# Attention with a learned position bias and experts, one core: pass 0 in steps of 128 rows of two heads

## What is computed

```python
def _attn_ref(q, k, v, w1, b1, w2):
    scores = scale * np.matmul(q, k.transpose(0, 1, 3, 2))
    ...
    psi_rel = np.log1p(np.abs(rel))
    psi_i = np.log1p(np.maximum(pos[:, None].astype(np.float32), 1.0))
    x = (psi_rel / psi_i)[..., None]
    h = np.maximum(x @ w1 + b1, 0.0)
    bias = h @ w2
    scores = scores + bias.transpose(2, 0, 1)[None, :, :, :]
    ...
    attn = attn / (np.sum(attn, axis=-1, keepdims=True) + 1e-09)
    return np.matmul(attn, v).astype(np.float32)

def _moe_ref(x, domain_probs, w1, w2):
    p = domain_probs / (domain_probs.sum(-1, keepdims=True) + 1e-09)
    for e in range(E):
        h = np.maximum(x @ w1[e], 0.0)
        out += p[:, e:e + 1] * (h @ w2[e])
```

## Time and profile before

| | us |
|---|---|
| median of 3 runs | 617.83 (616.99 to 619.96) |
| the profiled run | 619.55 |
| its span in the profile | 617.8 |
| PE busy | 581.8 (94%) |
| DVE busy | 295.9 (48%) |
| ACT busy | 262.8 (43%) |
| POOL busy | 121.1 (20%) |
| mean DMA rate | 117 GB/s |

### The profile page before, as it was taken

The page is one execution under the profiler, slowest core; times in us unless marked ns, Lnnn a source line. Parts: engine busy times, 40 slices in busy tenths (PEclk is TensorE's granted clock), DMA queues, the critical chain, the costliest instruction groups (busy, mean ns, idle before and its releaser), DMA issues.

```text
span 617.8 us, 9792 instructions
## 1 busy us (share of the span) xinstructions
PE 581.8 (94%) x3864; PEld 468.3 (76%) x3864; DVE 295.9 (48%) x608; ACT 262.8 (43%) x506; POOL 121.1 (20%) x176
## 2 busy tenths in 40 slices
PE   3857998969999999999999999999999999999997
PEld 1336665636677888878888788998899889989986
DVE  6935567578546534464345624361255226224511
ACT  4755566457536544454336534352045015303400
POOL 5144689100001131334313321000000000000000
PEclk9977999979999999999999999999999999999999
DMA  4882665366455543283164401241223114222201
GB/s 145 218 293 85 192 193 150 105 176 201 117 183 175 169 131 92 65 237 110 40 193 124 125 22 55 99 138 34 69 81 124 35 35 138 67 69 55 83 35 51
DMA packets 60654, 72.72 MB, mean 118 GB/s; under 512 B 23232, under 2 KB 39872, under 8 KB 60608
## 3 DMA queue, kind: packets, MB, share of 16 engines
q1 hardware_dynamic: 60416, 72.08, 38.9%
q10 hardware_dynamic: 192, 0.01, 0.0%
HBM read 59.10 MB, written 12.98 MB: 117 GB/s over the span
## 4 chain that ended last, share of the span: by engine, by line
PE 82%; DVE 5%; ACT 5%; DMA 3%; issue 2%; POOL 2%; ACTq 0%; DVEq 0%; POOLq 0%
PE m_bank L1130 12%; PE scores L1113 11%; PE x_bank L1130 11%; PE scores L1130 10%; PE m_bank L1113 9%; PE x_bank L1113 9%; PE turn L1061 4%; PE scores L1032 4%; PE scores L1092 4%; PE scores L1000 3%; PE turn L1000 2%; ACT probs L894 1%; PE turn L1065 1%; ACT w_hi L916 1%; DVE w_lo L761 1%
## 5 line engine op out<-in xcount | busy, mean ns | idle before, releaser
L654 POOL TENSOR_SCALAR probs<-probs,recip 128x576 f32<-128x576 f32 x72 | 53.9, 759 | 241.1 <-DVE recip L745 240.9
L761 DVE TENSOR_TENSOR w_lo<-w_raw,w_hi 128x1024 fp32r<-128x1024 f32 x64 | 80.1, 1252 | 25.2 <-ACT w_hi L916 25.2
L730 DVE CUSTOM_DVE_ANT_0 probs<-scores,bias 128x576 f32<-128x576 f32 x72 | 51.9, 754 | 53.6 <-PE scores L1032 39.6
L900 ACT COPY probs_t<-turn 128x512 f32<-128x512 f32 (+2 forms) x80 | 42.4, 551 | 79.9 <-PE turn L1061 79.0
L916 ACT CAST w_hi<-w_raw 128x1024 fp32r<-128x1024 f32 x64 | 66.5, 1045 | 3.2 <-DMA w_raw<-w_in 3.2
L894 ACT ACTIVATE probs<-probs,neg_max 128x576 f32<-128x576 f32 x72 | 55.4, 771 | 28.6 <-DVE neg_max L730 28.1
L1061 PE MATMUL turn<-ident,probs 128*128 128x128 f32 x288 | 46.1, 292 | 5.6 <-POOL probs L654 4.8
L1113 PE MATMUL scores<-x_hi,w_hi 128*128 128x256 f32 (+2 forms) x152 | 49.7, 327 | 0.9 <-DVE w_lo L761 0.7
L1113 PE MATMUL scores<-x_lo,w_hi 128*128 128x256 f32 (+2 forms) x152 | 48.9, 322 | 0.0
L1113 PE MATMUL scores<-x_hi,w_lo 128*128 128x256 f32 (+2 forms) x152 | 48.9, 322 | 0.0
L1061 PEld LDWEIGHTS turn<-ident,probs 128*128 128x128 f32 x288 | 34.0, 146 | 15.5 <-POOL probs L654 7.6
(11 more groups left out here) (142 smaller groups left out, 1245.6 us busy)
## 6 DMA issues: line engine op xcount, KB each, us to landing
w_raw<-w_in SPq DMA_DIRECT2D x64, 512.0 KB, 3.6
qk_raw<-qk_t_in SPq DMA_DIRECT2D x16, 576.0 KB, 4.8
bias<-bias_scratch SPq DMA_DIRECT2D x16, 576.0 KB, 4.9
v<-v_in SPq DMA_DIRECT2D x32, 128.0 KB, 3.4
bias_scratch<-probs SPq DMA_DIRECT2D x13, 288.0 KB, 4.3
bias_scratch<-probs_t SPq DMA_DIRECT2D x10, 288.0 KB, 3.0
bias_scratch<-rows SPq DMA_DIRECT2D x8, 288.0 KB, 4.2
out_dram<-acc SPq DMA_DIRECT2D x8, 256.0 KB, 2.0
```

The costliest lines, as they stand in the source:

```text
L654: pool.tensor_scalar(tile, tile, recip[:, stat(f, p, j)], 1.0, ALU.mult, ALU.mult).then_inc(normed, 1)
L730: dve.tensor_tensor_reduce(probs_of(f, p, j).rearrange("p (c j) -> p c j", c=2), score_of(f, j)[:, :, 0:HALF], bias_of(f, p, j).rearrange( ...
L761: dve.tensor_tensor(lo, raw, hi.bitcast(F32), ALU.subtract).then_inc(w_lo_out, 1)
L900: act.copy(sub_out(f, p, i), sub_in(n, i)).then_inc(out_act, 1)
```

## The change

It rewrites pass 0 in steps. `ORDER0` becomes the first rows of pairs 0 to 3, then the second rows of pairs 0 to 3, then pair by pair from pair 4 on. Each step has three turns of its own (`TURNS` 6 for a pair): one tile of each head and then the last 64 columns of both; the first and the third are copied by ACT, the second by DVE. Products and x follow each step, with 128 columns, one step behind its turns; x_hi stands one step behind the turns on ACT and x_lo two on DVE, and the two halves of `x_banks` take turns. Four pairs have places for q, k and v: places 2 and 3 of q and k lie in parts of `x_hi` and `x_lo` that pass 1 fills later, and v has `v_more`. The early bias sums use the turn bank and `x_banks`, and their ring `rows` and `probs_t`. The scores of step 0 stand on PE before the last two early bias sums. SP's list and POOL's splits are in another order. Pass 1 and the experts are as before. The diff is cut here; changes that only rename or count are left out.

```diff
-TURNS = (5, 7)
+TURNS = (6, 7)
+PLACES0 = 4
...
-ORDER0 = [(0, 0), (1, 0), (0, 1), (1, 1)] + [(p, t) for p in range(2, PAIRS) for t in range(2)]
+ORDER0 = [(p, t) for t in range(2) for p in range(4)] + [(p, t) for p in range(4, PAIRS) for t in range(2)]
...
-PART_T = ((0, 3), (3, JT))
-PRODUCTS_AT = {5: [(0, 0), (0, 1)], 6: [(1, 0)], 7: [(1, 1)],
-               **{2 * p + 4 + part: [(p, part)] for p in range(2, PAIRS - 2) for part in range(2)},
-               STEPS: [(PAIRS - 2, 0), (PAIRS - 2, 1)]}
-X_AT = {s + 1: p for s, parts in PRODUCTS_AT.items() for p, part in parts if part == 1}
...
-ACT_TURNS = ((0, 2, 4), (0, 1, 2, 3, 4, 5, 6))
+ACT_TURNS = ((0, 2, 3, 5), (0, 1, 2, 3, 4, 5, 6))
...
-            return score_bank[n % 2] if n < EARLY else (score_bank[0], turn_bank)[n % 2]
+            return (turn_bank, x_banks)[n % 2] if n < EARLY else (score_bank[0], turn_bank)[n % 2]
...
                 for n in range(EARLY):
                     store_rows(n)
                     if n in (1, 3):
-                        load_v(0, n // 2)
-                    if n in (5, 8):
-                        load_raw(2 + n // 8)
-                    if n == 11:
+                        load_raw(2 + n // 2)
+                    if n in (4, 5):
+                        load_v(0, n - 4)
+                    if n == 10:
                         rows_all_stored(EARLY // 2)
                         load_bias0(0, 0)
+                        load_bias0(1, 0)
                 rows_all_stored(EARLY)
...
                 for s in range(STEPS + 1):
                     if s >= 1:
                         normalise(0, *ORDER0[s - 1])
-                    if s >= 3:
-                        g = 3 + (s - 3) // 2
+                    g = 3 if s in (1, 2) else 4 + (s - 5) // 2
+                    if s in (1, 2) or s >= 5:
                         if s % 2:
                             high_of_qk(g)
                         else:
...
-                    if s in X_AT:
-                        low_of_x(0, X_AT[s])
+                    if s >= LAG + 2:
+                        low_of_x(0, *ORDER0[s - LAG - 2])
                     if s >= LAG:
                         p, t = ORDER0[s - LAG]
-                        take_turn(0, p, 2 * t + 1)
+                        take_turn(0, p, 3 * t + 1)
...
-                    if s in X_AT:
-                        high_of_x(0, X_AT[s])
-                    if s >= LAG and t == 1:
-                        take_turn(0, p, 4)
+                    if s >= LAG:
+                        take_turn(0, p, 3 * t + 2)
+                    if s >= LAG + 1:
+                        high_of_x(0, *ORDER0[s - LAG - 1])
...
+                    if f == 0 and i % 3 == 2:
+                        for side in range(2):
+                            mm = pe.transpose(bank[0:J_LAST, P * side:P * side + P],
+                                              probs_of(0, p, 2 * (i // 3) + side)[:, 4 * P:S], ident[:, :])
...
+                def step(s):
+
+                    if 1 <= s < STEPS:
                         score_step(0, *ORDER0[s])
-                    if s >= LAG and s != LAG + 2:
-                        turns_of_step(*ORDER0[s - LAG])
-                    for p, part in PRODUCTS_AT.get(s, ()):
-                        products(0, p, part)
+                    if LAG <= s < STEPS + LAG:
+                        p, t = ORDER0[s - LAG]
+                        turn(0, p, 3 * t)
+                        turn(0, p, 3 * t + 1)
+                        turn(0, p, 3 * t + 2)
+                    if s >= LAG + 1:
+                        products(0, *ORDER0[s - LAG - 1])
+
+                pe.wait_ge(w2_steps, 1 + G)
+                for n in range(EARLY):
+                    sum_block(n)
+                    if n == EARLY - 3:
+                        pe.wait_ge(eye_in, 16)
+                        pe.wait_ge(cleared, CLEARED)
+                        score_step(0, *ORDER0[0])
+                for s in range(1, STEPS + 1):
+                    step(s)
```

More of the change, by code:

```diff
@@ L83, in turn_order @@
     for p, t in ORDER0:
-        order += [(0, p, 2 * t), (0, p, 2 * t + 1)] + [(0, p, 4)] * t
+        order += [(0, p, 3 * t + i) for i in range(3)]
     return order + [(1, p, i) for p in range(PAIRS) for i in range(TURNS[1])]
@@ L130, with taken_by, x_n @@
 TAKEN = turn_taken()
-def taken_by(f, p):
-    upto = TAKEN[:max(turn_n(f, p, i) for i in range(TURNS[f])) + 1]
+def taken_by(f, p, i):
+    upto = TAKEN[:turn_n(f, p, i) + 1]
     return sum(a for a, _ in upto), sum(not a for a, _ in upto)
+def x_n(f, p, t=0):
+    return STEP_N[p, t] if f == 0 else STEPS + p
 def chunk_order():
@@ L287, in attention_and_experts @@
         raw_in = [sem(f"raw_in{r}") for r in range(2)]
-        v_in = [sem(f"v_in{r}") for r in range(2)]
+        v_in = [sem(f"v_in{r}") for r in range(PLACES0)]
         bias0_in = [[sem(f"bias0_in{r}_{t}") for t in range(2)] for r in range(2)]
@@ L310, in rows_of @@
             if n < EARLY:
-                return (rows, probs_2)[n // 4 % 2][:, n % 4, :]
+                if n % ROW_RING[0] < 4:
+                    return rows[:, n % 4, :]
+                half = probs_t[:, n % 4 // 2, 2 * (n % 2):2 * (n % 2) + 2, :]
+                return half.rearrange("p t q -> p (t q)")[:, 0:S]
             if n % ROW_RING[1] < 2:
@@ new lines, in _ @@
+                load_bias0(0, 1)
+                load_bias0(1, 1)
+                load_v(0, 2)
+                load_v(0, 3)
+                load_raw(4)
+                load_bias0(2, 0)
+                load_bias0(3, 0)
+                load_raw(5)
+                load_bias0(2, 1)
+                load_raw(6)
+                load_v(0, 4)
+                load_bias0(3, 1)
+                load_v(0, 5)
+                load_raw(7)
+                load_v(0, 6)
+                load_v(0, 7)
@@ L682, in _ @@
                 dve.memset(w2_block[:, :, :], 0.0).then_inc(w2_steps, 1)
-                dve.memset(v_sb[J_LAST:P, :, 4, :], 0.0).then_inc(cleared, 1)
+                for place in range(PLACES0):
+                    dve.memset(v_place(place)[J_LAST:P, :, 4, :], 0.0).then_inc(cleared, 1)
                 dve.memset(probs_t[J_LAST:P, :, 4, :], 0.0).then_inc(cleared, 1)
-                dve.memset(probs_t2[J_LAST:P, :, 4, :], 0.0).then_inc(cleared, 1)
+                dve.memset(probs_t2[J_LAST:P, :, :, 4, :], 0.0).then_inc(cleared, 1)
                 for q in (q_hi, q_lo):
@@ L714, in add_bias @@
                     if f == 0:
-                        if p >= 2:
-                            dve.wait_ge(turned, turn_n(0, p - 2, 4) + 1)
-                        elif p == 1 and j < 2:
-                            for rows_n in range(EARLY - STORES, EARLY):
-                                rows_are_stored(dve, rows_n)
+                        s = STEP_N[p, j // 2]
+                        if s >= 4:
+                            q, u = ORDER0[s - 4]
+                            dve.wait_ge(turned, turn_n(0, q, 3 * u + 2) + 1)
                         dve.wait_ge(bias0_in[p // 2 % 2][j // 2], 16 * (p // 4 + 1))
@@ L1087, in products @@
                     for c in range(chunks):
-                        for t in range(first_t, end_t):
+                        for k in range(JT):
                             for side in range(2):
                                 half = slice(D * side, D * side + D)
-                                dst = to[half, :, :] if f == 0 else to[half, c, :]
-                                mm = pe.matmul(dst, v_sb[:, 2 * (n % 2) + side, t, :],
-                                               probs_t_of(f, p)[:, side, t, cols * c:cols * c + cols],
-                                               start=t == 0, stop=t == JT - 1)
@@ L1095, in products @@
-                    if end_t == JT:
-                        mm.then_inc(weighed, 1)
+                                dst = to[half, :] if f == 0 else to[half, c, :]
+                                mm = pe.matmul(dst, values[:, side, k, :],
+                                               probs_t_of(f, p, t)[:, side, k, cols * c:cols * c + cols],
+                                               start=k == 0, stop=k == JT - 1)
+                    mm.then_inc(weighed, 1)
                 def hidden_part(ge, ft, c, first_k, end_k):
```

219 lines of the change are left out of this document (108 added, 111 removed).

## The result

The changed kernel takes **625.6 us** (median of 4 runs, 624.38 to 626.18), the kernel before beside it 618.53 (616.99 to 619.96). The ratio is 1.0108, with a 95% interval of 1.0085 to 1.0132: slower by 7.1 us, above the range of 614.3 to 623.5. The profiled run has 625.68 with a span of 623.9, that is 6.1 more than the span of before.

The account below looks back on a forecast made before the run. TensorE was taken as nearly the bound, so only moving pass 0's end pays. Bias -2.2, POOL and new steps +2.4, steps 4 to 15 -0.2, wait -0.2, end +1.3: about +1, hence 618.8 us, range 614.3 to 623.5.

Parts of the forecast that it names:

- First term, the bias load: Start of pass 0: earlier store of block 7 brings the bias tile at 36.8 instead of 39.0, gaining 2.2 us.
- the bias comes no earlier: Start: the queue holds the bias load until 39.0 and the POOL chain moves with it; 621.0 us, chance 0.08.
- Second term, steps 0 to 4: First attention steps: PE idles 3.0 us before step 3 for POOL's split; step 4 starts at 55.0, against 54.84.
- Third term, the steps: Steps 4 to 15: each takes 3.89 us instead of 3.7; eleven take 42.8 instead of 43.0.
- Fourth term, the end: End of pass 0: turns to first expert matmul take 5.7 us instead of 4.37, then 8.44 to the bias sum as before.
- products did shrink: Against the rival that product groups in the steps don't shrink as their columns do: 621.5 to 623.5 us, chance 0.18.
- turns did wait: Against the rival that the third turns in the steps don't wait for ACT: 4.5 us less, 614.3, chance 0.12.
- POOL was waited for: Against the rival that pair 3 is split before step 1 is normalised: 3.0 us less, 615.8, chance 0.12.

Follow-up runs that it names:

- run 1: Changed kernel with ScalarE casting the weight chunk ahead of the high part of x at the end of pass 0: 622.21 us, ratio 1.0052.
- run 3: Changed kernel with the third turn of each step behind the products instead of ahead of them: 621.38 us, ratio 1.0048.
- run 4: Changed kernel with 24 unused matmuls filling PE's idle time ahead of the first expert matmul: 625.14 us, ratio 1.0097.
- run 12: Changed kernel with only the first weight cast moved directly behind ACT's copy of step 14's first turn: 622.44 us, ratio 1.0055.
- run 5: Changed kernel with the first two loads of v moved behind the second pair of bias loads on SP: 623.22 us, ratio 1.0087.
- run 2: Changed kernel with pair 3's split on POOL moved ahead of the first normalisation, into the bias sums: 622.34 us, ratio 1.0046.
- run 11: Kernel before with pair 6's high part of x ahead of the first weight cast on ACT: 622.83 us, ratio 1.0069.
- run 6: Changed kernel with the edits of run 1, run 2 and run 3 together: 616.29 us, ratio 0.996.
- run 7: As run 6, with the first two v loads also moved behind the bias loads: 621.20 us, ratio 1.0031.
- run 8: As run 7, but pair 3's split stands after step 0's normalisation instead of in front: 617.82 us, ratio 0.9986.
- run 9: As run 6, with the weight cast directly behind the first turn's copy on ACT, ahead of the third turn's copy: 610.69 us, ratio 0.9889.
- run 10: As run 9, but pair 3's split stands between the normalisations of steps 0 and 1 instead of in front: 614.40 us, ratio 0.9941.

## Why the prediction was wrong, point by point

- **First term, the bias load: the step failed.** Forecast was a gain of 2.2, 27.5 from the first matmul to DVE's maxima. In the profiled run it is 30.1, 0.4 later than before, and in the other kernels with v in place and the split as changed (runs 1, 3, 4 and 12) 28.7 to 29.5, at best 1 earlier than the 29.7 of before. The failed step is the one from block 7's store to the tile: the load starts at 32.84 instead of at 31.5, and then takes 5.69 (put at 4.4 alone, 5.3 with a second load beside it). The issues of the v loads were put too low (3.8 on SP for the second, put at 1.7), but run 5 moves them away and the load still starts 23.4 behind the first matmul, so what holds it stays open. In the chain of waits of after it stands behind the store issued at 30.21. The rival "the bias comes no earlier" describes what happened.
- **Second term, steps 0 to 4: right in mechanism, too large by 0.8.** The wait for POOL is 3.12, forecast 3.0, and run 2, without it, takes 3.3 less. From the maxima to step 4 it is 17.4 instead of 18.2, because step 1's scores still ran at the full clock (0.40 for the first two, not 0.61), so that step 2 stands 2.80 behind step 1 and not 3.58. Step 4 at 55.91 looks close to the 55.0, but partly by luck: the first matmul was 0.8 earlier in this execution. Counted from it, step 4 is 1.7 later than forecast: 2.6 from the first term, less the 0.8 here.
- **Third term, the steps: right in mechanism, small by 0.08 a step.** Third turn idle 0.33 as forecast, 1.42 for the 1.37; the small transposes 0.31 for 0.27, products 1.24 for 1.26. That is 3.97 instead of 3.89, 0.8 over eleven steps. Run 3 shows that the wait and its copy cost 0.37 each step; it could have been avoided by order alone. The estimate of 1.62 from the Trainium skill's page "TensorE: Matmul & The Clock Gate", section "Back-to-back issue gap", does not hold here: 20 records of 128 columns take 1.24.
- **Fourth term, the end: this is where most is missing.** The step failed twice. From the turns to the expert matmul I had summed up to 6.2 and then chosen 5.7, with the argument that DVE's low part might be shorter than the 1.70 of the earlier trace rows. It became longer, 2.02, beside POOL's low parts of k and q, and the sum 6.49. Then I carried "8.44 as before" behind an idle stretch that had grown from 0.69 to 3.45. It took 10.91, since PE ran at the lower clock; where the clock stayed up it is 8.6 (runs 1, 4 and 12), so the sum of the instructions was nearly right and the clock was left out. Together 3.3 of the 5 that separate the forecast span from the measured one. Run 11 gets 6.47 and 10.01 from the kernel before. The 10.91 is the dearest case: in runs 2, 3 and 5 to 8, with the same idle time (3.43 to 3.53), it is 9.4 to 10.2.
- **The rest**: the bias sum was taken as the point from which all shifts carry unchanged. That holds for the kernel after (502.4 and 502.5), but by luck: the fourteen profiled executions have 502.2 to 503.8. The premise rested on a slip: in the earlier trace rows PE's ninth slice has 6 and its clock 7, and the 9s start with the tenth. In that slice lies the wait for the next weight chunk (5.7 idle before, 5.8 after), and how long the clock stays down behind it moves by over 1 us, which is an uncertainty of the method.
- **The rivals**: products did shrink, turns did wait, POOL was waited for. None of my rivals had a dearer tail, though the order of ACT shows plainly where it comes from: x behind the products, the cast behind x.

## What to carry to other kernels

When a step is moved between two engines' lists, follow what is queued behind it to the first long stretch of the next stage; here one small copy of x ahead of a weight cast cost 4.3 us by itself (run 11). Do not carry a duration of before across an idle stretch that has grown: behind 2.8 us more idle on PE the next nine matmuls took 4.18 instead of 2.3 (2.98 to 3.88 in runs 2, 3, 6 and 11). Of two edits that each help, one can lose its effect where they meet in one queue (run 6), so look at the chain again after each. Put the step that the next stage waits for directly behind the last thing that it needs. And before one profile's microsecond is put down to an edit, look at the same rows in runs that leave that place alone: the 1.2 of run 4 is in run 2 too.

## What the runs showed of the hardware that I had not expected

- Filling an idle stretch of 3.5 us with unused matmuls kept the clock up and saved 2.3 up to the bias sum; the median gained 0.5 to 1.1, within the uncertainty.
- The same idle stretch costs different amounts behind it. With 3.43 to 3.53 idle the way from the first expert matmul to the bias sum took 9.4 to 10.9. With the clock up it is 8.6 (runs 1, 4 and 12), and 8.0 where the third turn stands behind the products (runs 9 and 10). Behind the wait of some 5.7 the same 28 instructions (16 of a bias sum and 12 expert matmuls) took 4.2 to 5.7.
- DVE's fp32 subtraction of 128 by 1024 takes 1.24 or up to 2.04, and the difference goes with what POOL is in the middle of when it starts. With 0.93 left of POOL's low part of k (108.30 against 107.82 and 1.41) it takes 2.02; with 0.75 left, in run 3, 1.83; with 0.17 left, in run 11, 1.26. It is then POOL's next work that is longer: its low parts of q take 2.70 there, and 1.54 one step earlier in after. It looks as if each waits until the instruction of the other is through; that is a reading of these rows, which no run tests.
- A pair of v issues on SP took 1.54 in one place and 3.04 in another of the same run, 1.4 us apart, in after.
- What keeps the clock up in the same instructions in one execution and not in the next (run 6 against run 9, 2.0 us between the first matmul and step 4) stays open.
